# Splitting a sum of nine tiles between GpSimd and VectorE, with ScalarE placing the negated maximum (attention and two expert layers, float32, one core)

## The reference, cut to what matters

```python
q_pool = q.reshape(B, H, S // 2, 2, D).mean(axis=3)
scores = (1 / sqrt(D)) * q_pool @ k.T
scores = scores - max(scores, axis=-1)
attn = exp(scores)
attn = attn / (sum(attn, axis=-1) + 1e-9)
x = attn @ v
```

## Time and profile before

| | |
|---|---|
| median of 3 runs | 756.68 us (756.43 to 756.69) |
| the profiled execution | 756.79 us, its span 754.8 us |
| busy in the span | PE 97%, PEld 72%, DVE 64%, POOL 63%, ACT 52% |
| one head, from product to product | 13.72 us |
| granted TensorE clock, mean | 0.997 |

### The profile page before, as it was taken

The page is one execution under the profiler, slowest core; times in us unless marked ns, Lnnn a source line. Parts: engine busy times, 40 slices in busy tenths (PEclk is TensorE's granted clock), DMA queues, the critical chain, the costliest instruction groups (busy, mean ns, idle before and its releaser), DMA issues.

```text
span 754.8 us, 16897 instructions
## 1 busy us (share of the span) xinstructions
PE 730.2 (97%) x6404; PEld 545.3 (72%) x6404; DVE 480.5 (64%) x764; ACT 395.4 (52%) x784; POOL 477.2 (63%) x399
## 2 busy tenths in 40 slices
PE   4999999999999999999999999999999999999996
PEld 2777777776777777777777776533778888888885
DVE  7677676776776776767768746523895455454541
ACT  1566565664665655646656543313755454545452
POOL 1578878788788787887887873211784444444442
PEclk9999999999999999999999999999999999999999
DMA  3233334424425334344343208899401010101011
GB/s 101 67 91 80 104 104 135 121 90 135 118 89 149 106 105 147 93 137 117 99 133 113 79 26 311 314 388 367 162 1 43 0 43 0 42 0 42 1 42 43
DMA packets 51621, 81.82 MB, mean 108 GB/s; under 512 B 14556, under 2 KB 20572, under 8 KB 51548
## 3 DMA queue, kind: packets, MB, share of 16 engines
q1 hardware_dynamic: 51548, 80.83, 34.8%
HBM read 75.94 MB, written 4.79 MB: 107 GB/s over the span
## 4 chain that ended last, share of the span: by engine, by line
PE 86%; POOL 5%; DVE 4%; issue 2%; ACT 1%; DMA 1%; SPq 0%; POOLq 0%; DVEq 0%; ACTq 0%
PE ps L644 17%; PE ps L621 8%; PE ps L934 8%; PE ps L933 8%; PE ps L932 8%; PE ps L589 6%; PE ps L623 5%; PE ps L625 5%; PE ps L627 5%; POOL p_sum L483 4%; PE ps L655 3%; PE ps L554 2%; PE ps L820 2%; PE ps L922 2%; PE ps L846 2%
## 5 line engine op out<-in xcount | busy, mean ns | idle before, releaser
L483 POOL TENSOR_TENSOR p_sum<-p_sum,probs 128x576 f32<-128x576 f32 x158 | 234.7, 1485 | 23.2 <-ACT probs L1003 0.9
L1268 DVE TENSOR_REDUCE mx<-ps 128x2 f32<-128x1024 f32 (+1 forms) x160 | 189.4, 1218 | 81.7 <-PE ps L589 79.7
L1003 ACT ACTIVATE probs<-ps 128x576 f32<-128x576 f32 x288 | 183.8, 652 | 39.9 <-PE ps L627 26.0
L522 POOL TENSOR_TENSOR g_lo<-g_buf,g_hi 128x384 fp32r<-128x384 f32 x96 | 102.1, 1066 | 99.1 <-ACT g_hi L1164 99.1
L644 PE MATMUL ps<-probs,v_sb 128*64 128x288 f32 x1152 | 146.8, 409 | 0.1
L644 PEld LDWEIGHTS ps<-probs,v_sb 128*64 128x64 f32 x1152 | 79.9, 137 | 56.1 <-issue 5.2
L1497 DVE SCALAR_TENSOR_TENSOR v_buf<-u_buf 128x384 f32<-128x384 f32 x96 | 60.8, 634 | 87.3 <-ACT u_buf L1157 86.3
L932 PE MATMUL ps<-wo_hi,g_hi 128*128 128x512 f32 x288 | 112.9, 392 | 1.1 <-POOL g_lo L522 1.1
L934 PE MATMUL ps<-wo_lo,g_hi 128*128 128x512 f32 x288 | 113.1, 393 | 0.0
L933 PE MATMUL ps<-wo_hi,g_lo 128*128 128x512 f32 x288 | 112.9, 392 | 0.0
L1157 ACT ACTIVATE u_buf<-ps,half 128x384 f32<-128x384 f32 x96 | 55.6, 580 | 93.5 <-PE ps L922 93.5
(11 more groups left out here) (204 smaller groups left out, 1087.8 us busy)
## 6 DMA issues: line engine op xcount, KB each, us to landing
pre<-in_moe_w SPq DMA_DIRECT2D x41, 512.0 KB, 4.7
k_raw<-in_k SPq DMA_DIRECT2D x32, 288.0 KB, 3.9
v_sb<-in_v SPq DMA_DIRECT2D x32, 288.0 KB, 3.4
q_raw<-in_q SPq DMA_DIRECT2D x32, 256.0 KB, 2.6
from_x<-in_moe_w SPq DMA_DIRECT2D x9, 512.0 KB, 5.4
out<-o_stage SPq DMA_DIRECT2D x36, 128.0 KB, 2.3
p_inv<-inv_dram SPq DMA_DIRECT2D x62, 72.0 KB, 2.6
staged<-in_moe_w SPq DMA_DIRECT2D x8, 512.0 KB, 8.3
```

What stands on the lines that cost most here:

```text
L483: nc.gpsimd.tensor_tensor(total, total, probs[:, u, :], ALU.add).then_inc(probs_added, 1)
L1003: nc.scalar.activation(dst, ps[:, b0:b0 + 2, 0:HALF], ACT.Exp, scale=SCORE_SCALE).then_inc(exp_done, 1)
L1268: top = nc.vector.tensor_reduce(mx[0:w, NC * t:NC * t + 2], ps[0:w, b:b + 2, :], AX.X, ALU.max)
```

## The change

- GpSimd makes five adds of a head instead of six (tiles 8, 0, 1, 2, 3, 4). VectorE makes three instead of one: tile 7 += tile 6, tile 7 += tile 5, and, when GpSimd's last add is done, tile 7 += `p_sum`. The product with `ones` has one source, tile 7, so four matmuls instead of eight. The last head keeps its old scheme.
- The negated maximum is placed by ScalarE, in five copies scaled by a column mask `neg_mask`, behind the rounding of head `n + 2`. `h_mask`, its clearing and its two copies go.
- `low_k_q` becomes three pieces. The two small rests (`low_ends`) stand behind the new `add_total`.

```diff
-        ADDS = NT - 3
+        ADDS = NT - 4
+        TOP_ADDS = 3
...
                     if u == 0:
                         if n > 0:
-                            pool.wait_ge(sums_done, n)
+                            pool.wait_ge(pair_added, TOP_ADDS * n)
...
                 if n + 1 < HEADS:
-                    pe.wait_ge(probs_added, ADDS * n + ADDS)
-                    pe.wait_ge(pair_added, n + 1)
-                    for src, first in ((p_sum[:, :], True), (probs[:, NT - 2, :], False)):
-                        for c in range(4):
-                            mm = pe.matmul(ps[SLOTS * c:SLOTS * c + SLOTS, 4, HALF:HALF + QUAD], ones[:, 0:SLOTS],
-                                           src[:, QUAD * c:QUAD * c + QUAD], start=first, stop=not first)
+                    pe.wait_ge(pair_added, TOP_ADDS * n + TOP_ADDS)
+                    for c in range(4):
+                        mm = pe.matmul(ps[SLOTS * c:SLOTS * c + SLOTS, 4, HALF:HALF + QUAD], ones[:, 0:SLOTS],
+                                       probs[:, NT - 2, QUAD * c:QUAD * c + QUAD], start=True, stop=True)
...
-                        act.wait_ge(probs_added, ADDS * (n - 1) + (1 if s == 0 else (s + 1) // 2 * 2))
+                        act.wait_ge(probs_added, ADDS * (n - 1) + (1 if s == 0 else min((s + 1) // 2 * 2, ADDS)))
+                        if s >= NT - 4:
+                            act.wait_ge(pair_added, TOP_ADDS * n - 1)
...
+            def place_neg_max(m):
+                act.wait_ge(neg_full, m + 1)
+                r = D + QT
+                for t in range(QT):
+                    last = nc.scalar.activation(q_neg[m % 2][0:r, P * t:P * t + P], ps[0:r, neg_bank(m), 0:P], ACT.Copy,
+                                                scale=neg_mask[0:r, t:t + 1])
+                last.then_inc(neg_free, 1)
...
                 if n + 2 < HEADS:
                     round_k_q(n + 2)
+                if n + 1 < HEADS:
+                    place_neg_max(n + 1)
                 if n + 3 < HEADS:
                     double_q(n + 3)
...
-            def place_neg_max(m):
-                dve.wait_ge(neg_full, m + 1)
-                r = D + QT
-                nc.vector.tensor_tensor(q_neg[m % 2][0:r, :].rearrange("r (t c) -> r t c", t=QT),
-                                        ps[0:r, neg_bank(m), 0:P].unsqueeze(1).to_broadcast([r, QT, P]),
-                                        h_mask[0:r, :, :], ALU.mult).then_inc(neg_free, 1)
...
+                dve.wait_ge(pair_added, TOP_ADDS * n + 1)
+                nc.vector.tensor_tensor(probs[:, NT - 2, :], probs[:, NT - 2, :], probs[:, NT - 4, :],
+                                        ALU.add).then_inc(pair_added, 1)
+
+            def add_total(n):
+                dve.wait_ge(probs_added, ADDS * n + ADDS)
+                dve.wait_ge(pair_added, TOP_ADDS * n + 2)
+                nc.vector.tensor_tensor(probs[:, NT - 2, :], probs[:, NT - 2, :], p_sum[:, :],
+                                        ALU.add).then_inc(pair_added, 1)
...
                 if n + 1 < HEADS:
                     tops(n + 1, n > 0)
-                    place_neg_max(n + 1)
...
                 if n + 2 < HEADS:
-                    low_k_q(n + 2)
+                    low_k(n + 2)
+                    low_q(n + 2)
                 if n + 1 < HEADS:
                     add_pair(n)
+                    add_total(n)
...
+                if n + 2 < HEADS:
+                    low_ends(n + 2)
```

More of the change, by code:

```diff
@@ L152, in soft_moe_chain @@
     for name, n in (("ident", P), ("phi_sb", KD * SLOTS), ("sum_ident", SLOTS), ("fold", P), ("mx", QT * NC),
-                    ("ones", D), ("eps", 1), ("half", 1), ("l_neg", B + 1), ("all_neg", 1),
+                    ("ones", D), ("eps", 1), ("half", 1), ("neg_mask", QT), ("l_neg", B + 1), ("all_neg", 1),
                     ("row", P), ("ref_neg", 1), ("w_exp", B + 1), ("w_last", 1), ("e_sum", B + 1), ("e_mass", B + 1),
@@ L160, in soft_moe_chain @@
     ident, phi_sb, mx, half, ones, eps = (small[n] for n in ("ident", "phi_sb", "mx", "half", "ones", "eps"))
-    sum_ident, fold, l_neg, all_neg, row, ref_neg, w_exp, w_last, e_sum, e_mass, e_den, e_inv, c_top, c_sum, c_inv = (
-        small[n] for n in ("sum_ident", "fold", "l_neg", "all_neg", "row", "ref_neg", "w_exp", "w_last", "e_sum", "e_mass",
+    neg_mask, sum_ident, fold, l_neg, all_neg, row, ref_neg, w_exp, w_last, e_sum, e_mass, e_den, e_inv, c_top, c_sum, c_inv = (
+        small[n] for n in ("neg_mask", "sum_ident", "fold", "l_neg", "all_neg", "row", "ref_neg", "w_exp", "w_last", "e_sum", "e_mass",
                            "e_den", "e_inv", "c_top", "c_sum", "c_inv"))
@@ L650, in add_up @@
                 if n + 1 < HEADS:
-                    pe.wait_ge(probs_added, ADDS * n + ADDS)
-                    pe.wait_ge(pair_added, n + 1)
-                    for src, first in ((p_sum[:, :], True), (probs[:, NT - 2, :], False)):
-                        for c in range(4):
-                            mm = pe.matmul(ps[SLOTS * c:SLOTS * c + SLOTS, 4, HALF:HALF + QUAD], ones[:, 0:SLOTS],
-                                           src[:, QUAD * c:QUAD * c + QUAD], start=first, stop=not first)
+                    pe.wait_ge(pair_added, TOP_ADDS * n + TOP_ADDS)
+                    for c in range(4):
+                        mm = pe.matmul(ps[SLOTS * c:SLOTS * c + SLOTS, 4, HALF:HALF + QUAD], ones[:, 0:SLOTS],
+                                       probs[:, NT - 2, QUAD * c:QUAD * c + QUAD], start=True, stop=True)
                 else:
                     pe.wait_ge(probs_added, ADDS * n + LAST_ADDS)
-                    pe.wait_ge(pair_added, n + 3)
+                    pe.wait_ge(pair_added, TOP_ADDS * n + 3)
                     for src, first in ((p_sum[:, :], True), (p_rest[:, :], False)):
@@ L992, in exp_step @@
                     if s < NT - 2:
-                        act.wait_ge(probs_added, ADDS * (n - 1) + (1 if s == 0 else (s + 1) // 2 * 2))
+                        act.wait_ge(probs_added, ADDS * (n - 1) + (1 if s == 0 else min((s + 1) // 2 * 2, ADDS)))
+                        if s >= NT - 4:
+                            act.wait_ge(pair_added, TOP_ADDS * n - 1)
                     else:
-                        act.wait_ge(pair_added, n)
+                        act.wait_ge(pair_added, TOP_ADDS * n)
                         act.wait_ge(sums_done, n)
@@ L1034, in _ @@
             double_q(1)
+            act.wait_ge(consts_ready, 1)
+            place_neg_max(0)
+            act.wait_ge(zeroed, 1)
             round_k_q(1)
@@ L1240, in _ @@
                                   sum_ident[:, :].unsqueeze(1).to_broadcast([P, P // SLOTS, SLOTS]))
-            nc.vector.tensor_copy(h_mask[0:QT, :, :], ident[0:QT, 0:QT].unsqueeze(2).to_broadcast([QT, QT, P]))
-            nc.vector.tensor_copy(h_mask[D:D + QT, :, :],
-                                  ident[D:D + QT, D:D + QT].unsqueeze(2).to_broadcast([QT, QT, P])).then_inc(consts_ready, 1)
+            nc.vector.tensor_tensor(neg_mask[:, :], ident[:, 0:QT], ident[:, D:D + QT], ALU.add).then_inc(consts_ready, 1)
             dve.wait_ge(consts_ready, 1)
@@ L1247, in low, with low_k, low_q, low_ends @@
                 return nc.vector.tensor_tensor(dst, src, hi.bitcast(F32), ALU.subtract)
-            def low_k_q(m):
-                kh, kl, qh, ql, b = k_hi[m % 2], k_lo[m % 2], q_hi[m % 2], q_lo[m % 2], tail_bank(m)
+            def low_k(m):
                 dve.wait_ge(rounded, ROUNDS * m + 1)
-                low(kl[:, 0:KP], ps[:, 6, :], kh[:, 0:KP]).then_inc(turn_free, 1)
+                low(k_lo[m % 2][:, 0:KP], ps[:, 6, :], k_hi[m % 2][:, 0:KP]).then_inc(turn_free, 1)
+            def low_q(m):
                 dve.wait_ge(rounded, ROUNDS * m + 2)
-                low(ql[:, 0:P * QF], ps[:, 7, :], qh[:, 0:P * QF])
+                low(q_lo[m % 2][:, 0:P * QF], ps[:, 7, :], q_hi[m % 2][:, 0:P * QF])
+            def low_ends(m):
+                b = tail_bank(m)
                 dve.wait_ge(rounded, ROUNDS * m + ROUNDS)
-                low(kl[:, KP:KP + P], ps[:, b, 0:P], kh[:, KP:KP + P])
-                low(ql[:, P * QF:SQ], ps[:, b, P:P + QLAST], qh[:, P * QF:SQ]).then_inc(turn_free, 1)
+                low(k_lo[m % 2][:, KP:KP + P], ps[:, b, 0:P], k_hi[m % 2][:, KP:KP + P])
+                low(q_lo[m % 2][:, P * QF:SQ], ps[:, b, P:P + QLAST], q_hi[m % 2][:, P * QF:SQ]).then_inc(turn_free, 1)
             def top_of_rows(m, j):
@@ L1309, in add_last @@
                 for i, u in enumerate((NT - 3, NT - 2)):
-                    dve.wait_ge(pair_added, n + 1 + i)
+                    dve.wait_ge(pair_added, TOP_ADDS * n + 1 + i)
                     nc.vector.tensor_tensor(p_rest[:, :], p_rest[:, :], probs[:, u, :], ALU.add).then_inc(pair_added, 1)
@@ L1323, in tops @@
                 join_tops(m)
-            low_k_q(0)
+            low_k(0)
+            low_q(0)
+            low_ends(0)
             tops(0, False)
-            place_neg_max(0)
```

(5 more changed lines are left out.)

2 lines of the change are left out of this document (removed).

## The result

The changed kernel takes 782.27 us (median of 4 runs, 781.93 to 783.82) against 756.55 us beside it: ratio 1.0346, 95% interval 1.0334 to 1.0359. Its profiled execution has a span of 780.4 us, 25.6 more than before.

A forecast was written before the change was run, and what follows sets the result against it. TensorE's own list for each head was taken as the bound. 27 ordinary heads at 1.03 us, three late ones at 0.8 and head 30 at -0.5 made 28.1 on 756.79; forecast 784.8 us, range 768 to 790.

The forecast's parts named there:

- Who stands still: VectorE adds and GpSimd instructions reading SBUF exclude each other; the later stands still, making the ones products start 1.28 us late.
- The two rules: VectorE's end: GpSimd's end - 0.13 + own duration; GpSimd grows by VectorE's end - its own start - 0.14.
- The inverses for the division: Needed by GpSimd's first division half at 297.10; claimed there by 296.7, landing 2.6 us after issue at most.
- The start of the first add: VectorE's pair add was to start at 294.39, 0.10 us after GpSimd's fifth add, and so stand behind it.
- The late heads: Three heads with GpSimd's adds 0.28 us later; VectorE's pair add goes first, next head opens 0.48 late, 0.8 us each.
- TensorE's list: TensorE's work per head: four matmuls fewer in the ones products, 0.25 us a head given back.
- ScalarE's copies: Five copies of 69 x 128 placing the maximum, 1.35 us in ScalarE's idle time, costing nothing.
- The small rests: Two VectorE rests behind the third add; the next head's first product waits for them, just hidden, by under 0.1 us.
- The sum: 27 ordinary heads at 1.03 us, three late ones at 0.8 and -0.5 for head 30: together 28.1 us.
- Head 30: Has no rests, so its adds start early; 0.25 us for matmuls and about 0.25 for adds come back, -0.5.
- The first add going first: Rival: VectorE's pair add goes ahead of GpSimd's fifth add in most heads, 0.40 to 0.48 us a head, 769; chance 0.14.
- The faster case: Rival: TensorE's four matmuls go and VectorE's adds find room, the third ending before 297.61: 748 us; chance 0.05.

The follow-up runs named there:

- gate_divide: Changed kernel with GpSimd's two divisions held back by a wait until the three VectorE adds are through: 772.47 us, ratio 1.021.
- gate_all: Changed kernel with GpSimd's preparation and both divisions held back until the three adds are through, ScalarE's doubling moved behind its read of the sums: 758.92 us.
- pool_memset: Changed kernel with GpSimd's preparation and divisions replaced by clearings of the same tiles, that computation left out: 756.09 us, ratio 0.9995.
- early_gate: Changed kernel with VectorE adding tiles 4 and 5 early into its own buffer, GpSimd four adds, divisions held back until the adds are through: 747.41 us.
- place_only: Kernel before the change, with only the placing of the negated maximum moved to ScalarE as five scaled copies: 756.79 us, ratio 1.0004.
- pair_first: Changed kernel with the first of the three VectorE adds put ahead of the second large rest, same instructions and waits: 759.73 us, ratio 1.0046.
- no_total: Changed kernel without the third VectorE add, the ones product having two sources (eight matmuls) again: 757.23 us, ratio 1.0011.
- early_add: Changed kernel with VectorE adding tiles 4 and 5 early into its own buffer and GpSimd four adds, divisions not held back: 757.99 us, ratio 1.0021.
- place_on_vector: Changed kernel with the negated maximum placed by VectorE's masked product again, ahead of the rests, without ScalarE's five copies: 791.48 us, ratio 1.0461.
- ends_first: Changed kernel with the two small rests put ahead of the three VectorE adds again: 785.99 us, ratio 1.0388.

## Why the prediction was right

782.3 us was measured, 784.8 forecast, inside 768 to 790. Step by step:

- **Who stands still.** Right, and it carries the result. The two rules gave 1.9, 1.3 and 1.2 us for the adds (1.88, 1.30, 1.16), 1.37 for the preparation (1.38) and 1.19 for the first division (1.19). That the short GpSimd instructions count, which no row of before showed, is shown by gate_divide and gate_all, and that reading is what counts by pool_memset. The inverses for the division were there in time as well, though the 2.6 us of the earlier trace rows, which I took as the longest, is a median.
- **The start of the first add**, 0.10 behind the fifth: 0.14 in the head above. The late heads, forecast to open the next head 0.48 late, did so by 14.19 - 13.72 = 0.47.
- **TensorE's list.** 0.24 us a head came off (0.39 against 0.63). It is the gain that early_gate brings home.
- **ScalarE's copies**: 1.35 forecast, 1.39 measured, at no cost (place_only).
- **The small rests** in front of the next head: hidden in the sum, as forecast. TensorE's weight loads waited 6.8 us for them in all, 0.2 at most, beside the change-over.
- **The sum** was 28.1 us and came out as 25.6. An ordinary head cost 0.99, not 1.03 (-1.1). There were four late heads, not three (-0.6). Head 0 was dearer than counted by less than the others, since there are no divisions yet to lose a turn to (-0.5), and the start of the program came 0.2 later. Head 30, from which I expected -0.5, gave +0.1: its adds too start early only to stand still. The last 1.1 us came back behind the attention and have nothing to do with the sums: a stretch at the half clock that the change happened to avoid (below). That was luck and not forecast; without it the time would have been 783.4, still in the range. These terms make the 25.6.
- **The rivals.** The first add going first is real (the late heads, and pair_first by design at 759.7), but not in most heads. The faster case was right in its size, 748, and needed another distribution of the tiles: early_gate has 747.4.

## What to carry to other kernels

VectorE's and GpSimd's busy shares can't be added up as if they were independent. Where VectorE reads two SBUF tensors and GpSimd reads SBUF too, count turns, not microseconds of work: a 0.76 us add behind a GpSimd instruction costs that instruction's remainder too, and each short GpSimd instruction in between is one more turn. Look in the trace for one operation whose records have two lengths and set the long ones against the other engine's ends; the difference gives the rule, before anything is changed. Then put such adds where the other engine is quiet or only writes, or hold back the other's unhurried work by one wait. When a VectorE instruction is made cheaper or moved away just ahead of such an add, expect the freed time to turn into standing still (place_only).

## What the runs showed of the hardware that I had not expected

- **The clock at the start of the experts.** TensorE's granted clock before, around the stretch (columns: start:end, length, busy of PE, PEld, DVE, ACT, POOL, then the clock, DMA share, GB/s):

```profile
484.00:486.80 2.80, 2.11 (x20) 1.39 (x24) 1.39 (x7) 0.00 (x0) 0.63 (x1) 1.00 1.05 404
486.80:490.20 3.40, 3.40 (x21) 0.87 (x16) 0.00 (x0) 0.00 (x0) 0.00 (x0) 0.50 1.06 398
490.20:494.00 3.80, 3.80 (x40) 1.14 (x36) 0.00 (x0) 0.00 (x0) 0.00 (x0) 1.00 1.03 395
```

  In the changed kernel the same place has no such stretch:

```profile
510.50:513.60 3.10, 2.19 (x20) 1.39 (x24) 1.61 (x7) 0.00 (x0) 0.63 (x1) 1.00 1.05 405
513.60:517.00 3.40, 3.40 (x36) 1.04 (x32) 0.00 (x0) 0.00 (x0) 0.00 (x0) 1.00 1.06 396
```

  At 1.2 GHz 21 matmul records fit into 3.40 us, at 2.4 GHz 36. The same instructions stand there in both. From the last head's products with the values to the end the kernel before took 299.1 us and the changed one 298.0. TensorE's idle time ahead of this place is the same in both, two waits of 0.91 and 0.38 us for VectorE. So about 1.1 us hang on something that these rows do not show. The stretch is there in place_only, no_total, gate_divide, gate_all, pool_memset, early_gate and early_add as well; like the changed kernel, place_on_vector, ends_first and pair_first do without it. Comparisons across the two groups carry this 1.1 us.
- **The clock within the attention.** In place_on_vector it fell twice, each time behind a late head. In this one TensorE waited 2.01 us for the third add, and the next 3.4 us ran at half the clock:

```profile
201.81 0.45 PE L654 MATMUL ps<-probs,ones 128*32 128x144 f32 x8 [2.01 <-DVE probs L1316]
...
202.30:205.70 3.40, 3.40 (x26) 3.21 (x28) 1.61 (x2) 1.98 (x4) 0.12 (x1) 0.50 0.26 81
```

  The other two late heads waited 2.01 us as well, and the clock stayed at 2.4 GHz behind them. With waits of 1.2 us a head, as in the changed kernel, it stayed there throughout the attention.
- **The late heads.** In every seventh or eighth head one of GpSimd's adds starts 0.3 us late (four times in the changed kernel, 117 us apart), with nothing that it waits for in the trace: the exponential to which the profile puts that wait down had ended 0.37 before. What does it I did not find.
- **Who goes first when both begin together** is not told by the records. Within 0.01 us of each other either can: in early_add the preparation at 199.33 went ahead of the add at 199.32, and the add at 185.73 ahead of the preparation at 185.72. A kernel whose path runs through such a meeting, with further turns behind it, has heads of several lengths: 13.44 to 14.27 us in early_add.
